# Matmuls without a result in TensorE's waits, later constants on GpSimd, and another order of weight pieces and copies on ScalarE

## What is computed

```python
# recurrence, per head
m_new = max(f + m, i)
C = exp(f + m - m_new) * C + exp(i - m_new) * outer(v, k)
n = exp(f + m - m_new) * n + exp(i - m_new) * k
y = sigmoid(o) * (C @ q) / max(abs(n @ q), 1.0)

# experts: the (token, expert) pairs in falling order of logit
for idx in argsort(-(x @ w_gate).flatten()):
    # takes the pair if the token is free and the expert holds < 384
    ...
out[tokens of e] = relu(x[tokens of e] @ w1[e]) @ w2[e]

# second network
h = x @ w_in
y = (max(h, 0) + alpha * min(h, 0)) @ w_out
```

## Time and profile before

| | |
|---|---|
| time, median of 3 runs | 785.16 us (784.6 to 786.09) |
| time of the profiled execution | 785.32 us |
| its span | 783.2 us |
| busy: TensorE, VectorE, ScalarE, GpSimd | 734.6, 571.9, 322.7, 153.8 us |
| TensorE's granted clock, mean | 0.968 of full speed |
| DMA | 62.54 MB |

### The profile page before, as it was taken

The page is one execution under the profiler, slowest core; times in us unless marked ns, Lnnn a source line. Parts: engine busy times, 40 slices in busy tenths (PEclk is TensorE's granted clock), DMA queues, the critical chain, the costliest instruction groups (busy, mean ns, idle before and its releaser), DMA issues.

```text
span 783.2 us, 17825 instructions
## 1 busy us (share of the span) xinstructions
PE 734.6 (94%) x5911; PEld 689.5 (88%) x5911; DVE 571.9 (73%) x1458; ACT 322.7 (41%) x775; POOL 153.8 (20%) x246
## 2 busy tenths in 40 slices
PE   5999999853999999999999999999999999999994
PEld 4899999742989988998999899889989998999994
DVE  7778888977677868776877778677868777783442
ACT  5666777302234513532361245134413522361431
POOL 6367787401000110110011001101100110011001
PEclk9999999955899999999999999999999999999998
DMA  6888886104104100500320041005001400410000
GB/s 160 251 227 237 224 229 179 42 12 138 42 1 149 31 26 4 175 26 0 88 90 25 0 147 30 25 0 163 31 9 52 125 25 0 142 36 25 1 1 26
DMA packets 66781, 62.54 MB, mean 80 GB/s; under 512 B 35004, under 2 KB 57916, under 8 KB 66748
## 3 DMA queue, kind: packets, MB, share of 16 engines
q1 hardware_dynamic: 57016, 48.66, 21.8%
q0 software_dynamic: 2688, 8.65, 3.5%
q10 hardware_dynamic: 7044, 4.79, 2.0%
HBM read 53.43 MB, written 8.65 MB: 79 GB/s over the span
## 4 chain that ended last, share of the span: by engine, by line
PE 85%; DVE 6%; issue 3%; ACT 2%; DMA 1%; ACTq 1%; POOL 0%; SPq 0%; DVEq 0%
PE bank L924 21%; PE bank L930 18%; PE bank L929 18%; PE bank L948 5%; PE bank L949 4%; PE bank L800 4%; PE bank L783 2%; PE bank L751 2%; PE bank L734 2%; PE bank L974 1%; PE bank L839 1%; PE bank L973 1%; ACT decay L1079 1%; PE bank L848 1%; PE bank L918 1%
## 5 line engine op out<-in xcount | busy, mean ns | idle before, releaser
L924 PE MATMUL bank<-wo_hi,h_hi 128*128 128x320 f32 x384 | 120.6, 314 | 0.0
L930 PE MATMUL bank<-wo_hi,h_lo 128*128 128x320 f32 x384 | 118.6, 309 | 0.0
L929 PE MATMUL bank<-wo_lo,h_hi 128*128 128x320 f32 x384 | 118.0, 307 | 0.0
L1627 DVE SCALAR_TENSOR_TENSOR g_act<-g_neg,rest_alpha,bank 128x384 f32<-128x384 f32 x128 | 78.4, 613 | 40.2 <-ACT g_neg L1161 38.1
L658 POOL DMA_INDIRECT xe<-x_rows,idx_in x24 | 27.0, 1127 | 398.8 <-DVE idx_in L1565 357.7
L1161 ACT ACTIVATE g_neg<-bank 128x384 f32<-128x384 f32 x128 | 62.6, 489 | 94.9 <-PE bank L949 94.9
L1165 ACT CAST h_hi<-g_act 128x384 fp32r<-128x384 f32 x128 | 65.8, 514 | 83.7 <-DVE g_act L1627 83.2
L1159 ACT ACTIVATE h_hi<-bank 128x384 fp32r<-128x384 f32 x64 | 31.5, 492 | 162.3 <-PE bank L949 157.0
L924 PE MATMUL bank<-yT_hi,wi_hi 128*128 128x384 f32 x256 | 92.1, 360 | 0.0
L1632 DVE TENSOR_TENSOR h_lo<-g_act,h_hi 128x384 fp32r<-128x384 f32 x128 | 71.2, 556 | 26.2 <-ACT h_hi L1165 22.5
L929 PE MATMUL bank<-yT_lo,wi_hi 128*128 128x384 f32 x240 | 81.3, 339 | 0.0
(11 more groups left out here) (247 smaller groups left out, 1740.5 us busy)
## 6 DMA issues: line engine op xcount, KB each, us to landing
s<-w SPq DMA_DIRECT2D x8, 1024.0 KB, 5.2
s<-w SPq DMA_DIRECT2D x16, 480.0 KB, 7.2
s<-w SPq DMA_DIRECT2D x16, 256.0 KB, 6.0
k_in<-kT SPq DMA_DIRECT2D x48, 80.0 KB
q_in<-qT SPq DMA_DIRECT2D x48, 80.0 KB
k_row<-k SPq DMA_DIRECT2D x24, 160.0 KB, 3.4
v_in<-v SPq DMA_DIRECT2D x24, 160.0 KB, 3.9
gate_o<-o SPq DMA_DIRECT2D x24, 160.0 KB, 3.3
```

The lines of the kernel that those rows point to most:

```text
L924: pe.matmul(acc, ah, bh, start=start, stop=False, skip_group_check=True)
L929: pe.matmul(acc, ah, bl, start=False, stop=False, skip_group_check=True)
L930: return pe.matmul(acc, al, bh, start=False, stop=stop, skip_group_check=True)
L1627: dve.scalar_tensor_tensor(out=g_act[:, n, :], in0=g_neg[:, :], scalar=rest_alpha[:, j:j + 1], in1=acc, op0=ALU.mult, op1=ALU.add).then_in ...
```

## The change

- **Fillers.** `keep_busy(n, dst)` issues n matmuls of the f32 identity by itself, 128 columns, into a PSUM region whose content nobody reads afterwards: 14 before the gates are turned, 5, 2 and 2 around the router and turning work of the last two steps, 12 before the fetched rows of the first expert, 3 before each of the two later row groups, 2 after them.
- **Constants.** GpSimd's routing and search constants go from between the first tiles into the last chunk: search after the masks of tile 21, mask constants after tile 22, routing after tile 23. Waits on `consts` are renumbered.
- **ScalarE in chunks 1 to 4.** `high_piece` stands between the decays and `copy_xT`.
- **Gates.** ScalarE's decays wait for the copy of aT alone (`bias_ready`). VectorE splits the second group behind the probabilities of tile 1.
- **First expert.** The load of w1 comes in four DMAs with a semaphore for each of three parts, and ScalarE waits for each part by itself. The first hidden block is activated before the second third of w2 is rounded.
- **Matmuls.** In `down1` the matmul that adds up the counts stands one matmul earlier. In `up` the high product of the last 64 rows no longer waits for the low part of y.

```diff
+            def keep_busy(n, dst):
+
+                for _ in range(n):
+                    pe.matmul(dst[:, 0:P], ident[:, :], ident[:, :], start=True, stop=True)
+
+            keep_busy(14, XTB)
             turn_gates(0)
...
                 if isinstance(T, int) and T >= NT:
+                    keep_busy(5 if T == NT else 2, SCORE[0])
                     pe.wait_ge(out_read, NT)
                     pe.wait_ge(logit_read, T - 2)
                     router(*prev(c, b, 2))
+                if isinstance(T, int) and T == NT:
+                    keep_busy(2, SCORE[0])
...
-            pe.wait_ge(consts, 5)
+            pe.wait_ge(consts, 7)
...
+                keep_busy(12, UP[2])
                 for m in range(CT):
+                    if m:
+                        keep_busy(3, UP[2])
                     pe.wait_ge(first_rows[m], 16)
...
             turn_first()
+            keep_busy(2, UP[2])
```

```diff
             pool.sem_inc(prep_lo, 4)
-            weigh_values(0, 0)
-            routing_consts()
-            weigh_values(0, 1)
-            search_consts()
-            weigh_values(0, 2)
-            weigh_values(0, 3)
+            for b in range(B):
+                weigh_values(0, b)
...
             for b in range(1, B):
                 weigh_values(NCH - 1, b)
                 if b == 1:
+                    search_consts()
+                if b == 2:
                     mask_consts()
+            routing_consts()
             list_consts()
```

```diff
-                    act.wait_ge(gates_ready, c + 1)
+                    act.wait_ge(bias_ready, c + 1)
...
+                if weights:
+                    high_piece(c, b)
                 if not first(T, 1):
                     copy_xT(*((c, b - 1) if b else (c - 1, B - 1)))
...
-                    step(c, b)
-                    high_piece(c, b)
+                    step(c, b, weights=True)
...
             def high_w1(e, t):
-                if t == 0:
-                    act.wait_ge(stage1_in, 48 * e + 48)
+                act.wait_ge(stage1_in[t], 16 * e + 16 if t < 2 else 32 * e + 32)
...
             high_w2(0, 0)
+            activate(0, 0)
             high_w2(0, 1)
-            activate(0, 0)
             high_w2(0, 2)
```

```diff
-                sp.dma_start(s1[:, 0:2, :], w1[w, 0:2 * P, :].rearrange("(t p) f -> p t f", p=P)).then_inc(stage1_in, 16)
-                sp.dma_start(s1[0:REST, 2, :], w1[w, 2 * P:DM, :]).then_inc(stage1_in, 16)
-                sp.dma_start(s1[REST:P, 2, :], w1[w, 2 * P:DM, :]).then_inc(stage1_in, 16)
+                for t in range(2):
+                    sp.dma_start(s1[:, t, :], w1[w, P * t:P * t + P, :]).then_inc(stage1_in[t], 16)
+                sp.dma_start(s1[0:REST, 2, :], w1[w, 2 * P:DM, :]).then_inc(stage1_in[2], 16)
+                sp.dma_start(s1[REST:P, 2, :], w1[w, 2 * P:DM, :]).then_inc(stage1_in[2], 16)
...
                 for i, dst in ((0, aT), (2, wT), (1, gT)):
                     ins = dve.tensor_copy(dst[:, cs, :].rearrange("p c h -> p (c h)"), GATES[i][:, 0:n])
+                    if i == 0:
+                        ins.then_inc(bias_ready, len(GROUPS[g]))
...
                 if first(T, B):
+                    if b == 0:
+                        split_peak(1)
...
             gate_peaks(1)
-            split_peak(1)
```

```diff
                 pe.matmul(acc, ah, bl, start=False, stop=False, skip_group_check=True)
+                if between:
+                    add_four(*between)
                 return pe.matmul(acc, al, bh, start=False, stop=stop, skip_group_check=True)
...
                 if ready:
+                    pe.wait_ge(ready if highs is None else highs, count + 3)
+                pe.matmul(acc, wh[:, 2, js], ah[:, 2, :], start=False, stop=False, skip_group_check=True)
+                if highs is not None:
                     pe.wait_ge(ready, count + 3)
                 if ready is y_ready:
                     pe.wait_ge(y_twice, count // 3 + 1)
-                pe.matmul(acc, wh[:, 2, js], ah[:, 2, :], start=False, stop=False, skip_group_check=True)
...
-                        if route and j == J1 - 1 and t == 0:
-                            add_four(ph, J1 - 2)
```

More of the change, by code:

```diff
@@ L281, in build_program @@
         gates_ready = sem("gates_ready")
+        bias_ready = sem("bias_ready")
         qk_in = [sem(f"qk_in{b}") for b in range(B)]
@@ L322, in build_program @@
         token_sum = sem("token_sum")
-        stage1_in = sem("stage1_in")
+        stage1_in = [sem(f"stage1_in{t}") for t in range(3)]
         stage2_in = [sem(f"stage2_in{t}") for t in range(3)]
@@ L575, in routing_consts @@
                 pool.iota(route_tie[:, :, :], pattern=[[-8 * P, NCH], [-8 * S, B], [-1, E]], base=8 * 4095 + E - 1, channel_multiplier=-8,
-                          allow_small_or_imprecise_dtypes=True)
+                          allow_small_or_imprecise_dtypes=True).then_inc(consts, 1)
             def search_consts():
@@ L919, in turn_rows, with parts3 @@
                 ins.then_inc(xe_turned, 1)
-            def parts3(acc, a, b, start, stop, low=None):
+            def parts3(acc, a, b, start, stop, low=None, between=None):
                 (ah, al), (bh, bl) = a, b
@@ L970, in down1 @@
                             ins = parts3(ACC[t][:, 0:CAP], (w2_hi[:, j, ds], w2_lo[:, j, ds]),
-                                         (h_hi[:, j % 3, :], h_lo[:, j % 3, :]), j == 0, j == J1 - 1)
+                                         (h_hi[:, j % 3, :], h_lo[:, j % 3, :]), j == 0, j == J1 - 1,
+                                         between=(ph, J1 - 2) if route and j == J1 - 1 and t == 0 else None)
                         else:
@@ L1095, in copy_xT, with step @@
                 act.dma_start(x_rows_by_tile[c, b][:, DM:3 * P], x_sb[:, b % 2, 2 * P:DM]).then_inc(x_out[b % 2], 16)
-            def step(c, b):
+            def step(c, b, weights=False):
                 T = B * c + b
@@ L1351, in early_bests @@
                 ch = early
+                dve.wait_ge(consts, 7)
                 ch.link(dve.tensor_reduce(row_ones[:, :], ident[:, :].rearrange("p (c r) -> p r c", r=QR), X, ALU.add))
@@ L1587, in _ @@
             match_rows(ch, 0)
-            dve.wait_ge(consts, 7)
+            dve.wait_ge(consts, 8)
             own_list(ch, 0)
```

## The result

The changed kernel took 779.54 us (median of 4 runs, 779.31 to 780.74), the kernel before 785.48 us (4 runs, 784.6 to 786.09): ratio 0.9931, 95% interval 0.9917 to 0.9945 (the two medians by themselves give 0.9924). The forecast was 779.5. The profiled execution took 779.37 us, with a span of 777.6 us in place of 783.2. So 5.6 us left the span, and 0.35 us lay around it (2.12 us before, 1.77 after).

A forecast was written before the change was run, and what follows sets the result against it. TensorE was taken as the bound, with 85% of the chain, so only holes in its row and its own waits could pay. -2.4 -1.8 +0.4 -0.6 -1.4 = -5.8 us gave 779.5 us, range 776.0 to 782.8.

The forecast's parts named there:

- A: Start, up to the fades' matmuls: fillers, earlier decays, the later split and GpSimd's constants moved away save 2.4 us.
- B: Recurrence: moving the pieces of later weights on ScalarE removes the carried matmuls' delays at four places, saving 1.8 us.
- the second place: Recurrence, two tiles from 54.94 us: carried matmuls 0.33 us too late, a delay the moved piece would remove.
- C: Tail of the recurrence: VectorE's small instructions beside GpSimd's late constants and masks lose 0.4 us, between 0 and 1.5.
- D: First expert's weights and rows: split load, fillers and reordered activation save 0.6 us, between -1.6 and 2.0.
- E: Second network's takeover: a matmul needing only the high part fills a hole, 0.175 us for each of 8 experts, saving 1.4.
- second rival: Start and tail: engines sharing them absorb the gain, A stops at 1.1 and C costs 1.5; 781.9 us, chance 0.20.
- first rival: Search: the clock stays up, its 9 rounds gain 0 to 0.25 us each; 777.2 us, chance 0.12.
- third rival: Start and first expert: fillers never raise the clock, A gives 1.1 and D costs 1.6; 783.0 us, chance 0.06.
- the fourth: All filler groups: fillers cost far more than 0.45 us each and delay the transposes; 798 us, chance 0.04.

The follow-up runs named there:

- e6: Changed kernel with GpSimd's routing and search constants put back into the start; 779.93 us, ratio 0.9932 to the kernel before.
- e12: Changed kernel with VectorE's split of the second gate group put back before the probabilities of tile 1; 779.90 us, ratio 0.9926 to the kernel before.
- e4: Changed kernel without the nine fillers in the last two steps of the recurrence; 779.79 us, ratio 0.9923 to the kernel before.
- e1: Changed kernel without any fillers, all else kept; 781.05 us, ratio 0.9942 to the kernel before.
- e3: Changed kernel without the fillers around the first expert's rows; 780.69 us, ratio 0.9935 to the kernel before.
- e11: Changed kernel with GpSimd's routing constants moved to the head of the last chunk; 779.51 us, ratio 0.9922 to the kernel before.
- e10: Changed kernel with fillers in the first search's waits, three ahead of every later count; 782.55 us, ratio 0.9961 to the kernel before.
- e9: Changed kernel with fillers in the first search's waits, two ahead of every later count; 783.67 us, ratio 0.9974 to the kernel before.
- e8: Changed kernel with one filler ahead of each of the 9 counting rounds of the first search; 780.09 us, ratio 0.9938 to the kernel before.

## Why the prediction held, step by step

| step | forecast | profile | what the runs add |
|---|---|---|---|
| A, start | -2.4 | -2.22 | -1.5 to -1.6 in seven others with this start: the load of q is next |
| B, pieces | -1.8 | -1.67 | the piece's place 1.1 of it; the second place gave 0.03, not 0.33 |
| C, tail | +0.4 | +0.57 | 0.5 is the routing constants |
| D, first expert | -0.6 | -0.88 | fillers 0.5 to 0.7 of it |
| E, takeover | -1.4 | -1.39 | the wait alone 1.2 to 1.4 |
| sum | -5.8 | -5.6 | |

The signs and the order of size were right, and the reason was the one in the text: only holes in TensorE's row and its own waits could pay. E was the surest, because it came from one row times a count. **B** came from rows too, but not all of it as told: its four places gave 0.92, 0.03, 0.22 and 0.21 us, 1.4 in place of 1.8, and 0.3 from stretches outside them filled the gap. The wait at the second place is still there with the piece moved, so the piece's place was not its cause; what is, stays open.

The weakest step was **A**, and its number is in part luck. The sum followed VectorE's row alone up to the fades. The runs show that the load of q for the third tile is next, which the second rival had named ("because loads and GpSimd's masks are next"). In the profile of the changed kernel this load landed at 16.9; seven other kernels with the same start had F at 24.59 to 24.74, not 23.98 (an eighth at 24.14), and by them A is 1.5 to 1.6. The 1.2 us booked for VectorE without GpSimd's constants as neighbours come to 0.3 at F (e6), and the reordering of the split to nothing there (e12), both behind that load. The scores were not alone in holding up tile 0's probabilities, either: the row at 12.46 names ScalarE's decays, which ended at 12.40, just behind the scores at 12.31. That the fillers would run at 2.4 GHz for their last third came true in some profiles (from 5.8 us on in e4) and not in that of the changed kernel, where all ran at 1.2. There the transposes came 3.84 us behind the first scan, where 3.21 is usual (8.60 behind 5.39 before): 0.6 late, not 0.4.

In **D** the bound was named rightly (VectorE, and the load of w2), but the shares were not. The fillers gave 0.5 to 0.7 us, about what was booked for the whole term. Without them the split load and the reordered activation, for which 0.5 was named, left 0.1 (e1) and 0.3 (e3).

**C** was taken at 0.4 between 0 and 1.5; it is 0.57. It was read too simply. The product for x was said not to fit a lock, since it took 0.49 beside a mask. But that mask took 0.99 where others take 0.59; it ended 0.58 us behind the start of VectorE's next instruction, and so did the masks at this place in e6 (0.98 long) and e11 (0.87). So there GpSimd seems to have waited for the product. The rule of the Trainium skill (SBUF — State Buffer, "SBUF: two separate sides") says that whichever starts first holds the shared ports for the whole instruction, against a VectorE instruction with two SBUF inputs or one in a two-port mode; the prediction left the second kind out. With GpSimd second, the rows of the product agree. With GpSimd first, they agree for the one-input instructions (`isign`, the cast), though in which mode these ran no row shows, and not for those with two inputs: `scaled` started before the end of a mask (149.64, 149.86) in the kernel before and took 0.49 as always, and x, 0.1 us behind a mask's start in the changed kernel, took 0.56. The price that the prediction drew from the rule, 1.1 us more, did not come.

The first rival (the clock stays up through the search, 777.2 us) fell twice: the clock did not stay up, and e10 shows that it would have been worth 0.02 us a round. Its 0.25 us a round rested on the 24 matmuls at the lower clock, without asking whether VectorE's last comparison, which starts the last group of them, ends any sooner. The Trainium skill (TensorE: Matmul & The Clock Gate, "Why this matters for your kernels") spoke for it, by letting the clock fall only after a long idle gap; in the changed kernel it fell within 155 to 156 us, with no wait of TensorE above 1.5 us ahead of it, and in e9 once more at about 169.4 with no such wait at all, so the trace does not agree. The second rival was right about the loads; its 781.9 was too high, since its 1.5 us in the tail did not come and A did not stop at 1.1. The third rival fell with the scores at 1.16 us and the clock back at 187, the fourth with 0.44 us a filler.

## What to carry to other kernels

Filler matmuls pay only where dense work follows at once and TensorE itself is next on the path; where another engine sets the pace (the tail and the search here) a full clock is worth nothing, so ask first which engine ends each round. Search the waits of the bound engine for an instruction that needs only half of what is waited for: one such matmul in eight places gave a fifth of the whole gain. Cut profiles at events and compare piece by piece, and ask which wait ends last inside each piece: here one load that landed 0.7 us earlier passed for part of the result, and hid what other edits did.

## What the hardware showed that I had not expected

- The page prints a granted clock of 1.00 for the first 12 us in every kernel, yet a transpose there takes 0.44 us without fillers and 0.27 with them, and the fillers themselves 0.44 each where the clock is low. In that stretch durations tell the clock, not the column.
- The same 14 fillers, without a gap from 2.71 us on, saw the clock rise at very different times: their records go from 0.21 us apart to half of that at 5.8 us in e4, 6.7 in e10, 8.4 in e3, and not at all before their end (8.6) in the changed kernel and e9. At the rows and in the search it came up behind gapless work too: from 182.73 until between 186 and 187 in the changed kernel, from 156.6 until about 160 in e10 and until about 162.5 in e9. With TensorE 86% busy in short pieces (e8) it did not come up in 10 us.
- It fell within 152 to 153 us without the tail fillers (e1, e4), but within 155 to 156 in the kernel before, which has none either. With them it fell between 155 and 156 (changed, e9) and between 158 and 159 (e3, e8). In the changed kernel that is late enough for the last router's matmuls to run at the full clock, and nothing got faster.
- A running GpSimd mask of 0.59 us stretches VectorE's 0.24 us `isign` to 0.57, and one of 0.87 us a 0.17 us cast to 0.61, each ending about when the mask ends. Two-input instructions that started while one of these masks ran lost at most 0.07 us. The mask that started together with the two-input product for x took 0.87 to 0.99 us instead of 0.59.
